# Retention attention and two expert layers in one kernel: the first steps of the attention reordered, its value loads paired, and products of zeros added

## The reference

```python
# q, k, v: (8, 8, 576, 64)
scores = q @ k.T / sqrt(64)
gamma = 1 - 2 ** (-5 - h)                     # per head h
D = where(i >= j, gamma ** (i - j), 0)
x = (scores * D) @ v                          # no softmax
x = x.transpose(0, 2, 1, 3).reshape(4608, 512)
h = maximum(maximum(x @ w1, x @ w2), x @ w3)  # 512 -> 768
x = h @ w_out                                 # 768 -> 512
out = ((x @ u1) * (x @ u2)) @ u3 @ u_out      # 512 -> 1024 -> 1024 -> 512
```

## Time and profile before

| | |
|---|---|
| median of 3 runs | 1239.11 us (1238.57, 1239.11, 1243.99) |
| profiled execution, its time | 1238.84 us |
| its span (first to last instruction) | 1237.10 us |
| granted TensorE clock, mean | 1.000 |
| PE / PEld busy | 1220.1 / 1204.0 us |
| DVE / ACT / POOL busy | 769.9 / 486.5 / 432.9 us |
| DMA | 169.96 MB, mean 137 GB/s |

### The profile page before, as it was taken

The page is one execution under the profiler, slowest core; times in us unless marked ns, Lnnn a source line. Parts: engine busy times, 40 slices in busy tenths (PEclk is TensorE's granted clock), DMA queues, the critical chain, the costliest instruction groups (busy, mean ns, idle before and its releaser), DMA issues. The chain is left out here.

```text
span 1237.1 us, 21154 instructions
## 1 busy us (share of the span) xinstructions
PE 1220.1 (99%) x8288; PEld 1204.0 (97%) x8288; DVE 769.9 (62%) x1192; ACT 486.5 (39%) x779; POOL 432.9 (35%) x228
## 2 busy tenths in 40 slices
PE   7999999999999999999999999999999999999999
PEld 6999989999999999999999999999999999999998
DVE  6666857845546364658876767453535467776553
ACT  3433544523223232326655544242324234454441
POOL 3635528220200102052977761202020217266550
DMA  9999954120203011053464441213131342444441
GB/s 351 326 327 335 314 173 154 45 83 33 96 27 98 30 64 65 29 176 140 161 214 175 163 147 58 103 52 109 52 115 57 105 173 100 154 153 161 153 160 65
DMA packets 88084, 169.96 MB, mean 137 GB/s; under 512 B 9904, under 2 KB 59184, under 8 KB 87984
## 3 DMA queue, kind: packets, MB, share of 16 engines
q1 hardware_dynamic: 87984, 168.60, 39.0%
HBM read 106.70 MB, written 61.87 MB: 136 GB/s over the span
## 5 line engine op out<-in xcount | busy, mean ns | idle before, releaser
L1086 PE MATMUL ps<-chi,whi 128*128 128x384 f32 x2016 | 674.7, 335 | 5.3 <-DVE h L916 2.2
L1088 PE MATMUL ps<-chi,wlo 128*128 128x384 f32 x2016 | 673.5, 334 | 0.0
L1087 PE MATMUL ps<-clo,whi 128*128 128x384 f32 x2016 | 673.5, 334 | 0.0
L587 POOL TENSOR_TENSOR raw<-raw,raw 128x768 f32<-128x768 f32 (+2 forms) x96 | 264.0, 2770 | 590.9 <-DMA raw<-xd 203.3
L1086 PEld LDWEIGHTS ps<-chi,whi 128*128 128x128 f32 x2016 | 378.4, 188 | 8.9 <-DVE h L916 3.2
L1087 PEld LDWEIGHTS ps<-clo,whi 128*128 128x128 f32 x2016 | 378.4, 188 | 0.0
L1088 PEld LDWEIGHTS ps<-chi,wlo 128*128 128x128 f32 x2016 | 378.4, 188 | 0.0
L826 DVE TENSOR_TENSOR clo<-raw,chi 128x768 fp32r<-128x768 f32 (+2 forms) x168 | 256.0, 1552 | 32.8 <-ACT chi L749 32.7
L749 ACT CAST chi<-raw 128x768 fp32r<-128x768 f32 (+2 forms) x168 | 180.1, 1081 | 85.5 <-PE ps L1088 52.9
L817 ACT COPY w<-ps 128x384 f32<-128x384 f32 x126 | 60.7, 482 | 243.4 <-PE ps L1088 241.9
L804 ACT COPY u<-ps 128x384 f32<-128x384 f32 x126 | 60.8, 482 | 160.6 <-PE ps L1088 159.0
(11 more groups left out here) (43 smaller groups left out, 839.0 us busy)
## 6 DMA issues: line engine op xcount, KB each, us to landing
qks<-qk SPq DMA_DIRECT2D x32, 576.0 KB, 6.7
gd<-h SPq DMA_DIRECT2D x96, 192.0 KB, 1.9
raw<-gd SPq DMA_DIRECT2D x24, 768.0 KB, 6.0
hd<-h SPq DMA_DIRECT2D x72, 192.0 KB, 1.9
raw<-hd SPq DMA_DIRECT2D x24, 576.0 KB, 5.8
x2d<-h SPq DMA_DIRECT2D x48, 192.0 KB, 2.3
raw<-x2d SPq DMA_DIRECT2D x24, 384.0 KB, 4.5
outT<-h SPq DMA_DIRECT2D x48, 192.0 KB, 1.9
```

The source lines that it names most:

```text
L587: return nc.gpsimd.tensor_tensor(out_, a, b, op)
L1086: nc.tensor.matmul(to, w1, x1, start=(start and k == 0), stop=False, skip_group_check=True)
L1087: nc.tensor.matmul(to, w1, x2, start=False, stop=False, skip_group_check=True)
L1088: last = nc.tensor.matmul(to, w2, x1, start=False, stop=(k == KH[st] - 1), skip_group_check=True)
```

## The change

- PE does `sum_state` of step 2 ahead of `query_state`; all other steps keep their order. As the states of pairs 4 and 5 may now be made before those of 2 and 3 are read, there are four state buffers, and pairs 2 and 3 use the new ones (`state_buf`). The two new ones are zeroed too.
- Values of pairs 4 and up are loaded two pairs at a time, and tails two pairs at a time for all pairs; the tails have semaphores of their own, for which `values` waits on PE; `decay_values` no longer waits for a tail. The load of two pairs waits for `values` of both pairs that had the buffers. The tails of pairs 0 and 1 are issued behind the values of pair 3, those of 2 and 3 ahead of the values of 4 and 5.
- PE multiplies a zeroed tile `idle` (128 x 128 by 128 x 128) with itself, into banks that are not in use: 7 times before it waits for `zeroed`; in step 0, 4 times ahead of each `sum_state`, 4 times after that of pair 0, and 5 times after that of pair 1, once the state of pair 0 is made. DVE zeroes `idle` first of all.
- ACT's first instruction is a copy of one column of `idle`.

```diff
+def v_sem(n):
+    return n if n < 4 else (n - n % 2) % 6
+
+
+def v_count(n):
+    return 16 if n < 4 else 16 * (n // 6 + 1)
+
+
+def state_buf(n):
+    return n if n < 4 else n % 2
+
+
+
 U3_LOAD = {min(2 * kb + WC_FROM - 2, STEPS - 3): kb for kb in range(FT2)}
 U3_SPLIT = {min(2 * kb + WC_FROM - 1, STEPS - 2): kb for kb in range(FT2)}
 UO_LOAD = {1: (0, 1), 2: (2, 3)}
...
         o += 2 * NC * P * 4
         qdec = [at(f"qdec{i}", [P, NC, CH], f32, o + i * NC * CH * 4) for i in range(2)]
         o += 2 * NC * CH * 4
-        state = [at(f"state{i}", [P, NC, P], f32, o + i * NC * P * 4) for i in range(2)]
+        state = [at(f"state{i}", [P, NC, P], f32, o + i * NC * P * 4 if i < 2 else w_base[1] + (i - 2) * NC * P * 4)
+                 for i in range(4)]
         o += 2 * NC * P * 4
+        idle = at("idle", [P, CH + 2], f32, o); o += (CH + 2) * 4
         assert o <= 150528
         ps = ctx.enter_context(nc.psum_tensor("ps", [P, 8, 512], f32))
...
                 sp.dma_start(qks[n % 4][:, :], qk[n, :, :]).then_inc(qk_loaded[n % 4], 16)
             def load_v(n):
+                sp.dma_start(vs[:, n % 6, 0:NC * CH], vv[n, :, :]).then_inc(v_loaded[v_sem(n)], 16)
+
+            def load_two_v(m):
+                n = 2 * m
                 if n >= 6:
-                    sp.wait_ge(valued, n - 5)
-                sp.dma_start(vs[n % 6][:, 0:NC * CH], vv[n, :, :]).then_inc(v_loaded[n % 6], 16)
-                sp.dma_start(vs[n % 6][TAIL:P, NC * CH:], vt[n, :, :]).then_inc(v_loaded[n % 6], 16)
+                    sp.wait_ge(valued, n - 4)
+                sp.dma_start(vs[:, n % 6:n % 6 + 2, 0:NC * CH], vv[n:n + 2, :, :].rearrange("n p c -> p n c")
+                             ).then_inc(v_loaded[v_sem(n)], 16)
+
+            def load_tails(m):
+                n = 2 * m
+                sp.dma_start(vs[TAIL:P, n % 6:n % 6 + 2, NC * CH:], vt[n:n + 2, :, :].rearrange("n p c -> p n c")
+                             ).then_inc(vt_loaded[m % 3], 16)
             def load_k(n):
                 if n >= 2:
...
             load_decay(2, slice(4, HEADS))
             load_v(2)
             load_v(3)
+            load_tails(0)
             for m in range(STEPS):
                 if m in U3_LOAD:
                     load_u3(U3_LOAD[m])
...
                 for n in read_in(m):
                     if n >= PAIRS:
                         store_x(n)
-                for n in made_in(m + 2):
-                    load_v(n)
+                if m == 0:
+                    load_tails(1)
+                if 2 * m + 4 < NP:
+                    load_two_v(m + 2)
+                    load_tails(m + 2)
                 if m in WC_READ:
                     store_wc(WC_READ[m])
...
         def _(act):
             def decay_values(n):
                 p = n % PAIRS
-                act.wait_ge(v_loaded[n % 6], 32 * (n // 6 + 1))
+                act.wait_ge(v_loaded[v_sem(n)], v_count(n))
                 if n == 0:
                     act.wait_ge(vtab_loaded, 16)
                 if n >= 2:
...
                     act.wait_ge(prod, DONE[(last_of(tau - 1), USED_BY[pos])])
                 nc.scalar.copy(chi[st][pos][:, :, :], raw_block(tau, pos)[:, :, :]).then_inc(c_hi, 1)
+            act.wait_ge(idle_zeroed, 1)
+            nc.scalar.copy(idle[:, CH + 1:CH + 2], idle[:, CH:CH + 1])
             for n in made_in(0):
                 decay_values(n)
             for m in range(STEPS):
...
                 dve.wait_ge(c_hi, 7 * tau + pos + 1)
                 low(clo[st][pos][:, :, :], raw_block(tau, pos)[:, :, :], chi[st][pos][:, :, :]).then_inc(c_lo, 1)
+            nc.vector.memset(idle[:, :], 0.0).then_inc(idle_zeroed, 1)
             for i in range(4):
                 nc.vector.memset(probs[i][0:TAIL, :, NC * CH:SEQ], 0.0).then_inc(zeroed, 1)
-            for i in range(2):
+            for i in range(4):
                 nc.vector.memset(state[i][:, :, :], 0.0).then_inc(zeroed, 1)
             for i in range(6):
-                nc.vector.memset(vs[i][0:TAIL, NC * CH:], 0.0).then_inc(zeroed, 1)
-            dve.wait_ge(zeroed, 12)
+                nc.vector.memset(vs[0:TAIL, i, NC * CH:], 0.0).then_inc(zeroed, 1)
+            dve.wait_ge(zeroed, 14)
             for m in range(STEPS):
                 for n in made_in(m):
                     decay_scores(n)
...
                 pe.wait_ge(decayed, min(3 * (n - n % 2 + 2) + 2 * (n % 2 + 1), 3 * NP))
                 for c in range(1, NC + 1):
                     bank, cols = x_cols(n, c)
-                    last = nc.tensor.matmul(ps[:, bank, cols], state[n % 2][:, c - 1, :],
+                    last = nc.tensor.matmul(ps[:, bank, cols], state[state_buf(n)][:, c - 1, :],
                                             qdec[n % 2][:, c - 1, 0:min(CH, SEQ - c * CH)],
                                             start=(c == 1 or c == NC), stop=False, skip_group_check=True)
                 last.then_inc(queried, 1)
             def values(n):
                 pe.wait_ge(decayed, 3 * (n - n % 2 + 2))
+                pe.wait_ge(vt_loaded[n // 2 % 3], 16 * (n // 6 + 1))
                 for c in range(NC + 1):
                     bank, cols = x_cols(n, c)
                     for h in range(2):
                         own = slice(h * DH, h * DH + DH)
-                        last = nc.tensor.matmul(ps[own, bank, cols], vs[n % 6][:, c * P + h * DH:c * P + h * DH + DH],
+                        last = nc.tensor.matmul(ps[own, bank, cols], vs[:, n % 6, c * P + h * DH:c * P + h * DH + DH],
                                                 probs[n % 4][:, h, c * CH:min(SEQ, (c + 1) * CH)],
                                                 start=False, stop=(c >= NC - 1), skip_group_check=True)
                 last.then_inc(valued, 1)
...
                 if part == 3:
                     last.then_inc(wc_done, 1)
-            pe.wait_ge(zeroed, 12)
+
+            def run_idle(count, bank):
+                for _ in range(count):
+                    nc.tensor.matmul(ps[:, bank, 0:CH], idle[:, 0:CH], idle[:, 0:CH], start=True, stop=True,
+                                     skip_group_check=True)
+
+            pe.wait_ge(idle_zeroed, 1)
+            run_idle(7, S_WC)
+            pe.wait_ge(zeroed, 14)
             for m in range(STEPS):
                 for n in made_in(m):
                     scores(n)
                     if m == 0:
+                        run_idle(4, S_WC)
                         sum_state(n)
+                        if n == 0:
+                            run_idle(4, S_WC)
+                        else:
+                            pe.wait_ge(state_made, 2 * NC)
+                            run_idle(5, S_STATE)
                 for i in quarters(m):
                     wc_quarter(i)
+                for n in made_in(m) if m == 2 else ():
+                    sum_state(n)
                 for n in read_in(m):
                     query_state(n)
-                for n in made_in(m) if m else ():
+                for n in made_in(m) if m not in (0, 2) else ():
                     sum_state(n)
                 for n in read_in(m):
                     values(n)
```

More of the change, by code:

```diff
@@ L301, in build @@
         v_at = comb_base[B] + 4 * 6144
-        vs = [at(f"vs{i}", [P, V_COLS], f32, v_at + i * V_COLS * 4) for i in range(6)]
+        vs = at("vs", [P, 6, V_COLS], f32, v_at)
         ks = [at(f"ks{i}", [P, K_COLS], f32, (v_at + 6 * V_COLS * 4, o)[i]) for i in range(2)]
@@ L326, in sem @@
             return ctx.enter_context(nc.semaphore(name))
+        idle_zeroed = sem("idle_zeroed")
         zeroed = sem("zeroed")
         qk_loaded = [sem(f"qk_loaded{i}") for i in range(4)]
-        v_loaded = [sem(f"v_loaded{i}") for i in range(6)]
+        v_loaded = [sem(f"v_loaded{i}") for i in range(5)]
+        vt_loaded = [sem(f"vt_loaded{i}") for i in range(3)]
         k_loaded = [sem(f"k_loaded{i}") for i in range(2)]
@@ L692, in decay_values @@
                         vdec[n % 2][:, :, own],
-                        vs[n % 6][:, 0:NC * CH].rearrange("p (n c) -> p n c", c=P)[:, :, own],
+                        vs[:, n % 6, 0:NC * CH].rearrange("p (n c) -> p n c", c=P)[:, :, own],
                         mybir.ActivationFunctionType.Copy, scale=vtab[:, 2 * p + h:2 * p + h + 1]).then_inc(v_decayed, 1)
@@ L857, in make_state @@
                         if c == 0:
-                            nc.vector.tensor_copy(state[n % 2][own, c, own], new).then_inc(state_made, 1)
+                            nc.vector.tensor_copy(state[state_buf(n)][own, c, own], new).then_inc(state_made, 1)
                         else:
@@ L861, in make_state @@
                             nc.vector.scalar_tensor_tensor(
-                                state[n % 2][own, c, own], state[n % 2][own, c - 1, own], CHUNK_DECAY[2 * p + h], new,
-                                ALU.mult, ALU.add).then_inc(state_made, 1)
```

(2 more changed lines are left out.)

## The result

The changed kernel took 1243.13 us (median of 17 runs, 1241.63 to 1247.51), the kernel before 1239.25 in the same jobs (17 runs, 1237.65 to 1243.99). The ratio is 1.0032 with a 95% interval of [1.0024, 1.0041]: 3 to 5 us slower, 3.9 in the middle. That is within the 0.5% called "the same", and clear of noise. The profiled execution took 1242.21 us around a span of 1240.4, so 3.3 us more of span than before.

A forecast was written before the change was run, and what follows sets the result against it. TensorE was taken as the bound, dense from 40 us, so only that stretch's start could move. Step 2 ending 1.1 to 1.4 us later gave +1.3 on 1238.84, 1240.1; with a little for the clock, 1240.3, range 1237.8 to 1243.6.

The forecast's parts named there:

- the clock falls in the new wait: Step 2: some 3 us idle drops TensorE to 1.2 GHz, losing 1.9 to 3.4 us more; 1242.0 to 1243.6, chance 0.2.
- The loads are one full queue, and the keys land at 28.2 to 28.5 and 28.7 to 29.1 whatever their issue.: Step 2, keys of pairs 4 and 5: bytes ahead set their landing, so an earlier issue gains nothing.
- The paired loads cost nothing and bring nothing.: Value and tail loads: same bytes and big-load order; cost 0, with 0 to 0.6 us earlier allowed for what follows.
- the page's fixed cost: Some 2 us per load: merged value loads would bring the keys 2 us earlier, -1.1 instead of +1.3; rejected from the rows.
- The zeroing and the first scores 0 to 0.2 us late, seven products of zeros 1.7 to 3.6 us.: Kernel start: zeroing ends near 4.5 us, products by 4.7 at the latest, mostly covered by the first load.
- Step 1 ends between 1 us earlier and 1 later, and steps 0 and 1 drop out: Early steps: seventeen products against faster scores; the effect vanishes because step 2 waits for the keys anyway.
- some 3: Step 2: TensorE's idle time before the state sums, from about 25 to 28.3 us, where the hole was 1.14.
- The clock stays up (0.8): Step 2: TensorE keeps its upper clock through the new wait; the opposite case had chance 0.2.
- The wait costs 1.1 to 1.4: End of step 2: sums wait for keys and queries run after them, so the step ends 1.1 to 1.4 us later.
- All behind step 2 moves along one to one: After step 2: no wait from 40 us on could absorb the delay, so about 1.3 us reaches the end.
- keys in time: Step 2: a queue drained over 1.5 us faster lets the sums fill the hole; 1236.8 to 1238.1, chance 0.12.
- beyond 0.8 the gain must come from the queue too: Start of step 3: scores of pair 7 start at 33.3, their load lands at 32.5, which limits the gain.

The follow-up runs named there:

- f1: Changed kernel with the keys of pairs 4 and 5 issued ahead of the u3 and u_out weight blocks in step 1; 1239.43 us, ratio 0.9998.
- f4: Changed kernel with the keys of pairs 4 and 5 issued between the u3 block and the two u_out blocks in step 1; 1239.39 us, ratio 0.9995.
- f2: Changed kernel with the keys of pairs 4 and 5 issued behind the queries and keys of pairs 6 and 7; 1246.63 us, ratio 1.0050.
- e1: Changed kernel with the queries back ahead of the state sums in step 2, all other parts kept; 1240.20 us, ratio 1.0000.
- e4: Changed kernel without any products of zeros, memset and early ScalarE copy kept; 1242.44 us, ratio 1.0019.
- e2: Kernel before with only four state buffers and the state sums ahead of the queries in step 2; 1242.76 us, ratio 1.0022.
- e3: Changed kernel with 14 more products of zeros in step 2, ahead of the state sum of pair 4; 1242.18 us, ratio 1.0023.
- g1: e1 with 5 products of zeros as a plain delay ahead of the scores of step 3; 1242.23 us, ratio 1.0023 to the kernel before.
- g2: e1 with 14 products of zeros as a plain delay ahead of the scores of step 3; 1243.16 us, ratio 1.0030 to the kernel before.
- f3: Kernel before with the keys of pairs 4 and 5 issued ahead of the weight blocks in step 1; 1240.18 us, ratio 1.0007.

## Why the prediction was right, and where it was off

The forecast was 1240.3 us, the range 1237.8 to 1243.6; measured 1243.13. The sign, the place and the cause were right, the size was short by a factor of three: +1.3 forecast, +3.9 measured (3.0 to 5.1). What happened is the forecast and the rival "the clock falls in the new wait" together, 1242.0 to 1243.6, to which I gave 0.2. That the time lies in that rival's range is in part luck: the fall of the clock cost less than its 1.9 us at least, and about 1 us that neither of the two had came on top.

- *The loads are one full queue, and the keys land at 28.2 to 28.5 and 28.7 to 29.1 whatever their issue.* Right: 28.3 and 29.1, issued 1.9 us earlier. f1, f4 and f2 changed only their place in the queue, and the sums moved to 24.55, 25.90 and 31.87.
- *The paired loads cost nothing and bring nothing.* Nothing shows in e1. The sentence on the page's fixed cost hangs on this too: by the Trainium skill (DMA: Bandwidth & Descriptors, the section on the anatomy of one DMA) the keys would have come 2 us earlier, as an estimate; they did not. The estimate asked more of the page than it states: its fit is for single loads that GpSimd issues, and it puts most of the 2 us into the confirmation behind the last byte. That would be part of the lag of 2.3 to 2.4 us that the prediction found here, and not time in the queue; no run here takes the lag apart.
- *The zeroing and the first scores 0 to 0.2 us late, seven products of zeros 1.7 to 3.6 us.* Scores at 4.61 (4.51 before), products 3.34.
- *Step 1 ends between 1 us earlier and 1 later, and steps 0 and 1 drop out.* This step failed: step 1 ended 1.9 us earlier (21.42 against 23.29). The products of zeros brought the clock up by the first scores (1.16 us at 4.61), scores of pair 5 ended 1.9 us earlier, at 23.87, and the wait was 4.55 us, not "some 3". The start of the sums was indeed not moved, as e4 shows. But the wait got longer, and I had priced its length at nothing in the sum. No run shows that the length mattered: e2, with 2.16 us of it, lost its clock as well.
- *The clock stays up (0.8).* Wrong: the mean clock is lower in all 17 runs. The term was sized at 1.9 to 3.4 us if it came; by the profiles of changed and e3 it is 1.2 (sums and queries 4.40 us against 3.2). The longer wait is not what it took: in e2 it fell after 2.16 us. By the Trainium skill (TensorE: Matmul & The Clock Gate, Why this matters for your kernels) gaps are to be kept below about 3 us; here 2.2 us were already too long in e2, while 3.05 us were not in one execution of e4, so the page's figure is no safe limit for this kernel, and the measurement decides. I had taken "no row of before shows it" for evidence that it would hold.
- *The wait costs 1.1 to 1.4.* By the profiles without a fall of the clock 1.3 (e3) and 1.45 (e4) at step 3, by that of the changed kernel 2.8-1.2 = 1.6.
- *All behind step 2 moves along one to one.* Not shown, and doubtful: 1.3 at step 3 is 2.9 at the end in e3 and 1.3 of delay is 2.9 in g1, but 3.3 is 3.7 in g2, 1.45 is nothing in the profiled run of e4, which kept its clock, and the 1.4 us gained in f1 are 0.3 (-0.9 to 1.4). About 1 us of the 3.9 is in this. What makes it stays open; the late waits of the attention and the idle time of the expert layers differ from profile to profile by 1 to 2 us, and a single profile of each can't tell whether the delay causes them.
- *The rival "keys in time"* did not come by itself, but f1 made it so, and it gave no gain over the kernel before, less than the 1236.8 to 1238.1 that I had for it: "beyond 0.8 the gain must come from the queue too" was right, and even the 0.8 is not seen.

## What to carry to other kernels

Before an instruction is moved into an idle gap, look up when each of its operands lands, not only what its engine waited for. The move here filled 1.1 us on paper, but the keys had just come in time for the old place. When the loads are one full queue, as here, a landing is the bytes ahead divided by the rate, plus the lag (2.3 to 2.4 us here); an issue 1.9 us earlier did not change it, another place in the queue did. So the loads must be reordered together with the work, and what is pushed back by it must be looked up too (here the weight blocks, ScalarE's conversions and its copies of X). A quicker start ahead of such a load was worth nothing here.

## What was not expected of the hardware

- Products of zeros count as work for the clock. With seven of them from 1.05 to 4.39 us the first scores run at 1.16 us for sixteen records in the changed kernel and f4, at 1.43 and 1.79 in e1 and e3, where the rise comes during them, and still at 2.08 in f1, f2, g1 and g2, where it comes behind them (by 6.9 us, in f2 by 11.3). In the profiles without products of zeros the first scores take 2.08 us everywhere.
- TensorE's clock fell after 2.16 us of idle time (e2) and within 2.27 (e1), but not in the profiled execution of e4 after 3.05 us. The same kernel has both: 10 of 12 runs of e4 have a lower mean clock. The length of the gap alone doesn't decide. The mean granted clock is no full record: the profile before has 1.00 in its first stretches, where scores take 2.08 us, the time of the lower level; in the profile of f3 the same 2.08 us at 13.24 us stand under a granted clock of 0.50.
- A load issued into the full queue lands 2.3 to 2.4 us behind the moment at which its bytes are through: 26.1 to 28.45 and 22.8 to 25.25 in the kernel before.
